# Six token tiles of 504 and 496 columns in place of five of 512 and one of 448

## The reference, cut to what it computes

```python
qn = q / (norm(q, axis=1) + 1e-06);  kn = k / (norm(k, axis=1) + 1e-06)   # norms over the tokens
s = kn.transpose(0, 2, 1) @ qn / tau                  # 256 x 256 per batch
a = softmax(s, axis=-1)
x = (v @ a).reshape(12032, 256)
h = x @ w_in                                          # w_in 256 x 2048
g = maximum(h, 0) + alpha * minimum(h, 0)
y = g @ w_out                                         # w_out 2048 x 256
```

## Time and profile before

| | |
|---|---|
| median of three runs | 1076.69 us |
| profiled execution, its own time | 1076.63 us |
| its span, first to last instruction | 1074.8 us |
| granted TensorE clock, mean | 1.000 |
| TensorE matmuls | 1070.9 us busy, 4995 |
| VectorE | 847.0 us busy |
| ScalarE | 654.6 us busy |
| GpSimd | 40.4 us busy |
| DMA, mean over the span | 74 GB/s |

### The profile page before, as it was taken

How to read it: one execution, slowest core, us unless ns; L and a number is a source line. 1 busy time by engine, 2 the same in 40 slices (tenths; PEclk the granted TensorE clock), 3 DMA queues, 4 the chain that set the end, 5 groups by cost and what they waited for, 6 DMA issues and landing times.

```text
span 1074.8 us, 13902 instructions
## 1 busy us (share of the span) xinstructions
PE 1070.9 (100%) x4995; PEld 906.2 (84%) x4995; DVE 847.0 (79%) x1349; ACT 654.6 (61%) x1100; POOL 40.4 (4%) x54
## 2 busy tenths in 40 slices
PE   9999999999999999999999999999999999999998
PEld 7888888888888888888998888888888888888898
DVE  6999987877877777787798887777777777787776
ACT  6676677667766555655666655555555555555544
POOL 0000000000000000000000000000000000000000
PEclk9999999999999999999999999999999999999999
DMA  9621154455453102103212101201202202200101
GB/s 382 284 88 50 40 158 127 138 160 150 134 162 99 30 13 54 45 9 79 69 30 73 50 11 49 59 8 52 59 1 59 59 0 54 57 1 10 40 1 35
DMA packets 30837, 80.07 MB, mean 74 GB/s; under 512 B 2992, under 2 KB 9264, under 8 KB 29232
## 3 DMA queue, kind: packets, MB, share of 16 engines
q1 hardware_dynamic: 24288, 67.80, 18.1%
q0 software_dynamic: 6336, 11.28, 6.8%
q10 hardware_dynamic: 144, 0.11, 0.0%
HBM read 64.04 MB, written 12.32 MB: 71 GB/s over the span
## 4 chain that ended last, share of the span: by engine, by line
PE 100%; ACT 0%; issue 0%; POOL 0%; POOLq 0%
PE y_ps L538 47%; PE x_ps L512 24%; PE z_ps L512 12%; PE p_ps L512 6%; PE x_ps L444 4%; PE s_ps L464 3%; PE p_ps L498 2%; PE s_ps L444 1%; PE y_ps L498 1%; PE y_ps L553 0%; PE z_ps L440 0%; PE p_ps L486 0%; PE p_ps L473 0%; PE p_ps L479 0%; ACT y_stage L876 0%; PE s_ps L435 0%
## 5 line engine op out<-in xcount | busy, mean ns | idle before, releaser
L538 PE MATMUL y_ps<-g_hi,w_hi 128*128 128x512 f32 (+1 forms) x760 | 293.1, 386 | 0.0
L538 PE MATMUL y_ps<-g_hi,w_lo 128*128 128x512 f32 (+1 forms) x760 | 292.9, 385 | 0.0
L538 PE MATMUL y_ps<-g_lo,w_hi 128*128 128x512 f32 (+1 forms) x760 | 292.9, 385 | 0.0
L757 ACT CAST g_hi<-h 128x512 fp32r<-128x512 f32 (+1 forms) x384 | 234.0, 610 | 78.6 <-DVE h L1011 69.3
L1011 DVE SCALAR_TENSOR_TENSOR h<-h,small_sb 128x512 f32<-128x512 f32 (+1 forms) x384 | 273.7, 733 | 0.0
L1003 DVE SCALAR_TENSOR_TENSOR h<-z_ps,sigma_neg,h 128x512 f32<-128x512 f32 (+1 forms) x192 | 141.7, 738 | 148.0 <-ACT h L747 147.6
L1045 DVE TENSOR_TENSOR g_lo<-h,g_hi 128x512 fp32r<-128x512 f32 (+1 forms) x384 | 249.9, 670 | 0.8 <-ACT g_hi L757 0.5
L747 ACT ACTIVATE h<-x_ps,sigma_neg 128x512 f32<-128x512 f32 (+1 forms) x192 | 130.7, 681 | 175.2 <-PE x_ps L512 165.1
L747 ACT ACTIVATE h<-x_ps,sigma 128x512 f32<-128x512 f32 (+1 forms) x192 | 130.6, 680 | 124.8 <-PE x_ps L512 120.2
L538 PEld LDWEIGHTS y_ps<-g_hi,w_hi 128*128 128x128 f32 x760 | 142.7, 188 | 27.3 <-issue 0.3
L538 PEld LDWEIGHTS y_ps<-g_hi,w_lo 128*128 128x128 f32 x760 | 142.7, 188 | 27.0
(11 more groups left out here) (129 smaller groups left out, 1009.4 us busy)
## 6 DMA issues: line engine op xcount, KB each, us to landing
rows_t<-qk_t SPq DMA_DIRECT2D x32, 376.0 KB, 4.0
stage<-qk SPq DMA_DIRECT2D x10, 1024.0 KB, 13.3
v_stage<-v_t SPq DMA_DIRECT2D x20, 512.0 KB, 4.6
y_t<-y_stage SPq DMA_DIRECT2D x20, 512.0 KB, 2.8
pair<-qk SPq DMA_DIRECT2D x19, 512.0 KB, 3.7
v_stage<-v_t POOLq DMA_DIRECT2D x27, 256.0 KB, 4.1
scratch<-w_in SPq DMA_DIRECT2D x12, 256.0 KB, 2.8
v_stage<-v_stage POOLq DMA_DIRECT2D x9, 256.0 KB, 3.3
```

What stands on the lines that cost most here:

```text
L538: product = nc.tensor.matmul(y_ps[t][oc][:, 0:H], w_part[:, j, ws], g_part[:, k, 0:H], start=jp == 0 and k < 2 and w_part is w_hi and g_pa ...
L757: nc.scalar.copy(g_hi[:, k, 0:H], h[:, k, 0:H]).then_inc(g_hi_ready, 1)
```

## The change

It computes the same result with the same number of tiles, groups and instructions. `half_width` is read from a list: N / 16 = 376 units of 8 tokens are dealt to six tiles, so `WIDTHS` is 504, 504, 504, 504, 496, 496. The columns of a batch stay 3008 (before: 5 x 512 + 448). The token offset of a tile within its batch is the sum of the widths before it. Buffers keep their 512 columns, of which 504 or 496 are used. In `mix_first_v` the first tile's sums are cut to its width.

```diff
+    UNIT = 8
+    assert N % (2 * UNIT) == 0
+    WIDTHS = [UNIT * (N // (2 * UNIT) // TILES + (t < N // (2 * UNIT) % TILES)) for t in range(TILES)]
+    assert 2 * sum(WIDTHS) == N and max(WIDTHS) <= HALF
+
     def half_width(T):
-        t = T % TILES
-        return HALF if t < TILES - 1 else (N - 2 * HALF * (TILES - 1)) // 2
+        return WIDTHS[T % TILES]
+
+    def token_in_batch(T):
+        return 2 * sum(WIDTHS[:T % TILES])
 
     def first_token(T):
-        return T // TILES * N + T % TILES * 2 * HALF
+        return T // TILES * N + token_in_batch(T)
...
             def load_v(T):
-                b, t = T // TILES, T % TILES
+                b = T // TILES
                 H = half_width(T)
...
-                n0 = t * 2 * HALF
+                n0 = token_in_batch(T)
...
             for T in range(1, ALL):
-                b, t = T // TILES, T % TILES
+                b = T // TILES
                 H = half_width(T)
-                n0 = t * 2 * HALF
+                n0 = token_in_batch(T)
...
             def mix_first_v(what):
-                b11, b12, b21, b22 = (v_stage[:, n, :] for n in range(4))
+                b11, b12, b21, b22 = (v_stage[:, n, 0:half_width(0)] for n in range(4))
```

## The result

The changed kernel takes 1087.06 us, median of six runs (1086.82 to 1087.35), against 1076.68 us of six runs before. The ratio is 1.0097 with a 95% interval of 1.0087 to 1.0106: slower by 10.4 us. The forecast was 1086.3 us. The profiled execution took 1087.07 us, with a span of 1085.3.

A forecast was written before the change was run, and what follows sets the result against it. TensorE's gapless matmul stream bounds the kernel, count times pitch. 1076.63 us, +9.8 for 16.05 ns overhead at the new widths, -0.1 for the ends, gives 1086.3 us; own range 1082 to 1090, full range 1074.2 to 1097.

The forecast's parts named there:

- The bound: Whole kernel: a gapless stream of TensorE matmuls; time is their number times the pitch, the distance between two starts.
- The overhead o: Each matmul's time beyond its columns at 2.4 GHz; taken as 16.05 ns at 504 and 496 columns, giving +9.8 us.
- The edges and covers: Tile edges mixing two widths, and VectorE and ScalarE work hidden under matmuls: both costed at nothing.
- The reason given for o: TensorE streams whose width is not 256 or 512 pay extra, as 448 did at 16.05 ns over 180 matmuls.
- Rival (c): TensorE matmuls: only 448 was slow; 504 and 496 run with 512's 13.33 ns overhead, 1074.6 us; chance 0.27.
- (d): TensorE matmuls: overhead on a straight line from 448 to 512, 13.67 and 14.0 ns, 1076.6 us; chance 0.13.
- (b): TensorE matmuls: odd widths never settle, overhead 18.3 ns, 1096.1 us, up to 1103 at 20.0; chance 0.20.
- ScalarE, the transfers and the waits: Beside the matmuls: ScalarE's busy sum within 2 us, transfers cost nothing, TensorE's waits stay below 2 us.
- VectorE's busy sum: VectorE's work over the kernel: linear in columns, so its sum was to stay within 2 us.
- The chain: The chain that ended last: to stay 100% TensorE.
- wrong in its ground: Stated sign of failure: a wait of VectorE or a transfer on the chain, or a granted clock below 1.00.

## Why the prediction was right

The bound: right. The time is the number of matmuls times their pitch in both kernels. From the start of tile 7 to the end the pitches leave nothing over: 336 positions of tile 10 at -3.33 ns, then 24 at -3.33 and 360 at +20.6 (496 for 448), are +6.2 us, and the trace has 414.2 for 408.0 us.

The overhead o at 504 and 496, the term on which all hung: taken as 16.05 ns from tile 11, measured 16.67 at both. That is 0.72 x 6 x 0.62 = 2.7 us too little.

The edges and covers, costed at nothing, are what makes up for it: 1.9 us. The first group starts at 56.68 in place of 57.01 us (0.3, within what the other kernels' heads differ, 56.3 to 57.5). Tiles 0 to 3 last 359.31 us in place of 359.97 although 504 runs at the pitch of 512, for the most part since a group with twelve 256-column matmuls takes 11.64 us for 11.66 or a little more. Tiles 4 to 6 have 5.27 us more where the pitches give 6.22; there the twelve matmuls of `make_m` add 1.45 us to a group of 496 and added 1.52 to one of 448, 0.4 us over six groups; the rest of the 0.95 isn't traced. So 12.4 - 1.9 = 10.5 us. The sum was good to 0.8 us because two misses of 2.7 and 1.9 had opposite signs: that much is luck, and the 0.3 us at the start is chance between executions.

The reason given for o was only half right. That one width has several pitches, by what ran before, is shown (488: 220.0 and 225.5). That widths other than 256 and 512 pay is not: 384 pays nothing beyond 13.3, and 512 itself pays 20 from column 8 on. What decides is how the moving operand and the weights lie against each other within 64 columns, and the width comes in together with it. That 448's 16.05 came so near the 16.67 of 504 and 496 is luck as well: in the table the overheads between 448 and 502 columns go from 14.0 (502) to 22.2 (488). Rival (c), an overhead of 13.3 close to 512, fell by 504 itself; (d), a straight line with 13.67 and 14.0, by the 16.67 at both widths; (b)'s 18 to 20 ns is what some stretches show (498 columns have 19.2), but not these tiles.

ScalarE, the transfers and the waits: nearly as forecast. The prediction counts 1152 products of `up`; these are the `up` matmuls into X, of 2016 in all. TensorE's weight loads waited 0.8 us for ScalarE, a transfer cost one wait of 0.5 us. VectorE's busy sum grew by 2.7 us, a little over the 2 us allowed, off the path. The chain is 96% TensorE, not 100, by its first 60 us. By its own words the prediction would be wrong in its ground if VectorE or a transfer stood on the chain, and both now do; yet that stretch ends 0.3 us earlier than before, so nothing of the 10.4 us comes from there, and the ground holds.

What stays open is the mechanism. The runs show that the pitch depends on how weights and moving columns lie against each other, with a period of 64 columns, and on what ran before, for the 60 matmuls of a stretch; they don't show what inside the chip does it, nor why 504, 506, 510 and 512 columns share a pitch.

## What to carry to other kernels

Where TensorE's stream has no gaps, read its pitch from start to start, for each width and from stretches of hundreds of matmuls: equal tiles are not cheaper tiles, and a width is worth only what its own pitch says. Ask of each row whether it comes from a settled stretch or from one behind another shape, and keep both as bounds. A bare stream of the same instructions, many widths in one kernel, gives the table, but where the pitch depends on what ran before, the last word is the full kernel's.

## What the runs showed of the hardware that was not expected

- fp32r matmuls back to back, from 264 columns up and with both operands at column 0, have 10 to 22 ns over their columns at 2.4 GHz, and not on a line: 504, 506, 510 and 512 columns take 226.7 ns, 502 take 223.2, 498 take 226.7.
- Weights and moving operand interact: 512 columns take 226.7 ns with both at column 0 or both at column 8, and 233.3 with one of them shifted by 8.
- The pitch keeps a memory of what ran before: 488 columns settle at 220.0 ns behind 504 and at 225.5 behind 512, to the end of stretches of 60.
- fp32r matmuls with weights of 128 columns didn't come closer than about 111.5 ns: 240 columns take 112.0, 128 take 111.7.
- bf16 doesn't have the overhead: 504 columns take 212.4 ns, and 496, 448 and 256 also 2.5 over their columns. Shifted starts were not run in bf16.
